# The first expert's w1 split moved into the last router unit, the second w2 load queued behind the first gather, and the first rows split bank by bank

## What is computed

```python
x = attention(q, k, v, cap)              # 4 batches, 12 heads, 448 rows, 64 columns, tanh-capped scores
x = square(relu(x @ w_in)) @ w_out       # 1792 x 768, inner width 2048
# a mixture of 8 experts, each of capacity 224 tokens
logits = x @ w_gate                      # 1792 x 8
order = argsort(-logits.flatten())       # greedy: the best (token, expert) pairs first
for idx in order:                        # a pair is taken if the token is free and the expert not full
    tok, e = idx // 8, idx % 8
    ...
for e in range(8):
    h = maximum(x[assigned == e] @ w1[e], 0)      # w1[e]: 768 x 1024
    out[assigned == e] = h @ w2[e]                # w2[e]: 1024 x 768
```

## Time and profile before

| what | value |
|---|---|
| median of 3 runs | 1215.44 us (1215.41 to 1217.42) |
| the profiled execution | 1214.78 us, its span 1213.0 us |
| PE busy | 1110.7 us, 92% of the span |
| DVE busy | 832.2 us, 69% |
| ACT busy | 623.8 us, 51% |
| POOL busy | 212.3 us, 17% |
| PE's mean granted clock | 0.944 of full speed |

### The profile page before, as it was taken

One profiled execution on the slowest core, in us unless ns is written; L12 is line 12 of the kernel. 1 busy time (PEld: TensorE's weight loads), 2 busy tenths in 40 slices (PEclk: granted clock), 3 DMA queues, 4 the chain that ended last, 5 costly groups with the idle time before them and its releaser, 6 DMA issues.

```text
span 1213.0 us, 25561 instructions
## 1 busy us (share of the span) xinstructions
PE 1110.7 (92%) x9795; PEld 905.9 (75%) x9795; DVE 832.2 (69%) x1741; ACT 623.8 (51%) x977; POOL 212.3 (17%) x345
## 2 busy tenths in 40 slices
PE   6999988999998999999967999999994599999997
PEld 6974434444443999999966999999994588888885
DVE  3159998999999366666574455555556589898972
ACT  1268876999996233333343111111135387878872
POOL 0025444454453000000000000000000022222201
PEclk7569998999999999999987999999996799999999
DMA  7017311111110000000150000000336456666501
GB/s 262 16 50 186 104 45 46 45 54 59 53 31 16 1 2 1 2 2 1 41 170 2 24 25 25 24 2 24 128 128 224 157 213 249 234 247 240 209 24 46
DMA packets 54644, 103.46 MB, mean 85 GB/s; under 512 B 3872, under 2 KB 32288, under 8 KB 54560
## 3 DMA queue, kind: packets, MB, share of 16 engines
q1 hardware_dynamic: 52000, 91.26, 22.2%
q0 software_dynamic: 2560, 11.01, 2.9%
HBM read 91.25 MB, written 11.01 MB: 84 GB/s over the span
## 4 chain that ended last, share of the span: by engine, by line
PE 68%; DVE 15%; ACT 7%; issue 6%; POOL 1%; DMA 1%; DVEq 0%; ACTq 0%; SPq 0%; POOLq 0%
PE psum L1278 17%; PE psum L1319 15%; PE psum L1438 6%; PE psum L1424 6%; PE psum L1204 5%; PE psum L1218 4%; PE psum L1229 4%; PE psum L1188 3%; DVE arena L1116 2%; ACT arena L694 2%; DVE arena L840 2%; PE psum L1362 2%; PE psum L1181 2%; DVE arena L1110 2%; ACT arena L599 2%
## 5 line engine op out<-in xcount | busy, mean ns | idle before, releaser
L1319 PE MATMUL psum<-arena 128*128 128x224 f16 x2304 | 243.2, 261 | 18.1 <-DVE arena L804 18.1
L1319 PEld LDWEIGHTS psum<-arena 128*128 128x128 f16 x2304 | 215.5, 99 | 22.2 <-DVE arena L804 19.0
L1278 PE MATMUL psum<-arena 128*128 128x224 f16 x2304 | 223.3, 259 | 0.0
L1278 PEld LDWEIGHTS psum<-arena 128*128 128x128 f16 x2304 | 220.2, 98 | 2.0 <-ACT arena L616 1.1
L476 POOL TENSOR_SCALAR arena<-arena 112x448 f32<-112x448 f32 x192 | 121.8, 647 | 191.6 <-DVE arena L830 191.6
L599 ACT ACTIVATE arena<-arena 112x448 f32<-112x448 f32 x192 | 143.6, 751 | 4.3 <-DVE arena L842 4.1
L1229 PEld LDWEIGHTS psum<-arena 112*112 112x112 f32 x768 | 74.3, 135 | 87.0 <-POOL arena L476 56.0
L1424 PE MATMUL psum<-arena 128*128 128x224 f16 x1152 | 116.5, 266 | 16.0 <-DVE arena L1124 16.0
L1424 PEld LDWEIGHTS psum<-arena 128*128 128x128 f16 x1152 | 112.9, 100 | 19.8 <-issue 14.1
L1438 PE MATMUL psum<-arena 128*112 128x384 f16 x768 | 127.1, 326 | 0.4 <-issue 0.4
L590 ACT ACTIVATE arena<-psum,arena 112x896 f32<-112x896 f32 x96 | 96.5, 1005 | 51.5 <-PE psum L1204 50.6
(11 more groups left out here) (207 smaller groups left out, 1273.0 us busy)
## 6 DMA issues: line engine op xcount, KB each, us to landing
arena<-moe_w SPq DMA_DIRECT2D x16, 3072.0 KB, 13.4
arena<-moe_w_out SPq DMA_DIRECT2D x32, 384.0 KB, 4.1
arena<-moe_w_in SPq DMA_DIRECT2D x16, 384.0 KB, 5.2
arena<-q SPq DMA_DIRECT2D x24, 224.0 KB, 2.9
arena<-k SPq DMA_DIRECT2D x24, 224.0 KB, 3.1
arena<-v SPq DMA_DIRECT2D x24, 224.0 KB, 2.7
y_rows<-arena SPq DMA_DIRECT2D x16, 336.0 KB, 3.2
arena<-y_rows,arena POOLq DMA_INDIRECT x16, 4.6
```

The lines of the kernel that those rows point to most:

```text
L1278: last = pe.matmul(out, w_split[:, f, z, k * 128:(k + 1) * 128], x[u % 2][:, k, :], start=(k == 0 and m == 0), stop=(k == KD - 1 and m == 2))
L1319: last = pe.matmul(out, w_split[:, k, z, m * 128:(m + 1) * 128], g[u][:, k, :], start=(k == 0 and j == 0), stop=(k == KF - 1 and j == 2))
```

## The change

Five things are done; the first three are one piece.

1. The sums of absolute values of w1 of expert 0 (ACT, four instructions) stand in unit 6, between `y_evict(6, 0)` and `yT_evict(6, 1)`, instead of at the start of unit 7. The scale is made by DVE in the first round of the last router phase.
2. At the start of unit 7 ACT makes the four quarters of the high half.
3. POOL makes the low half: for each quarter a multiplication of the staged float32 words by the scale, in place, and a subtraction of the float16 high half, written as float16.
4. SP waits for the first gather to land before it issues the load of w2 of expert 1.
5. In the tail between unit 7 and the experts, PE ranks before it transposes the last block; DVE makes the small tables before the large one, and the large one in two halves, with PE's product following half by half; `turn_rows` signals each bank; and for expert 0 ACT and DVE split the rows bank by bank. ACT's sums of w2 of expert 0 come ahead of that, right behind the last unit. `gather_rows(e)` and the later experts' wait count three signals for each expert where they counted one.

```diff
             load_w(1, 0, s_w1l, s_w1L, w1p, KD)
+            sp.wait_ge(s_ygl, 32)
+            sp.sem_inc(s_sp, 1)
             load_w(1, 1, s_w2l, s_w2L, w2p, KE)
...
             pool.partition_all_reduce(w1_tops, w1_sums, 128, RMAX).then_inc(s_wt, 1)
+            for j in range(4):
+                quarter = slice(j * EW // 4, (j + 1) * EW // 4)
+                hold(s_w1H, j + 1)
+                stage = stage_part(0, j * EW // 4, EW // 4)
+                pool.tensor_scalar(stage, stage, w1_scl, 1.0, ALU.mult, ALU.mult).then_inc(s_w1s, 1)
+                hold(s_w1s, j + 1)
+                pool.tensor_tensor(w1L[:, quarter], stage, w1H[:, quarter], ALU.subtract).then_inc(s_w1L, 1)
             hold(s_ym, NU)
...
             for u in range(NU):
                 if u == NU - 1:
-                    act.wait_ge(s_w1l, 16)
-                    act.wait_ge(s_ym, NU - 1)
+                    act.wait_ge(s_we1, 3)
                     for j in range(4):
-                        wait(act, s_ws, j)
-                        act.activation(abs_out, stage_part(0, j * EW // 4, EW // 4), ACT.Abs, accum_out=w1_sums[:, j:j + 1]).then_inc(s_ws, 1)
+                        quarter = slice(j * EW // 4, (j + 1) * EW // 4)
+                        act.activation(w1H[:, quarter], stage_part(0, j * EW // 4, EW // 4), ACT.Copy, scale=w1_scl).then_inc(s_w1H, 1)
                 yT_evict(u, 0)
...
                 y_evict(u, 0)
+                if u == NU - 2:
+                    act.wait_ge(s_w1l, 16)
+                    act.wait_ge(s_ym, NU - 2)
+                    for j in range(4):
+                        wait(act, s_ws, j)
+                        act.activation(abs_out, stage_part(0, j * EW // 4, EW // 4), ACT.Abs, accum_out=w1_sums[:, j:j + 1]).then_inc(s_ws, 1)
                 yT_evict(u, 1)
...
-                w1_hi(0)
-                w1_hi(1)
+                if not first(e + 2):
+                    w1_hi(0)
+                    w1_hi(1)
                 rows_out(1)
...
-                w1_hi(2)
                 if first(e + 2):
-                    w1_hi(3)
+                    act.wait_ge(s_ym, NU)
                     for j in range(4):
                         w2_abs(e + 2, j)
-                if expert_live(e + 2):
-                    wait(act, s_tT, e + 3)
+                    ygH_banks = ygH.rearrange("p (b n) -> p b n", b=3)
+                    act.wait_ge(s_we1, 4)
+                    for b in range(2):
+                        act.wait_ge(s_tT, b + 1)
+                        act.activation(ygH_banks[:, b], psum[:, BANK_ET + b, 0:2 * CAP], ACT.Copy, scale=y2_scl).then_inc(s_ygB, 1)
+                    act.wait_ge(s_tT, 3)
+                    act.activation(ygH_banks[:, 2], psum[:, BANK_ET + 2, 0:2 * CAP], ACT.Copy, scale=y2_scl).then_inc(s_ygH, 1)
+                else:
+                    w1_hi(2)
+                if expert_live(e + 2) and not first(e + 2):
+                    wait(act, s_tT, 3 * (e + 3))
...
                     if r > 0:
                         read_count()
+                    elif phase == E - 2:
+                        dve.wait_ge(s_wt, 1)
+                        dve.tensor_reduce(w1_amax, w1_tops, AX.X, ALU.max).then_inc(s_wa1, 1)
+                        dve.wait_ge(s_wa1, 1)
+                        pow2_scale(dve, w1_amax, w1_inv, w1_scl, s_we1, 0)
...
-            dve.tensor_tensor(low_hot[0:TP], low_of[0:TP].unsqueeze(2).broadcast_to([TP, CH, TP]),
-                              lows[0:TP].unsqueeze(1).broadcast_to([TP, CH, TP]), ALU.is_equal).then_inc(s_hot, 1)
...
             dve.tensor_tensor(group_tok[0:TP], group_hot[0:TP], tok[0:TP].unsqueeze(2).broadcast_to([TP, CH, CH]), ALU.mult).then_inc(s_hot, 1)
+            for h in range(2):
+                half = slice(h * CH // 2, (h + 1) * CH // 2)
+                dve.tensor_tensor(low_hot[0:TP, half], low_of[0:TP, half].unsqueeze(2).broadcast_to([TP, CH // 2, TP]),
+                                  lows[0:TP].unsqueeze(1).broadcast_to([TP, CH // 2, TP]), ALU.is_equal).then_inc(s_hot, 1)
...
+                    if first(e):
+                        ygL_banks, ygH_banks = (y.rearrange("p (b n) -> p b n", b=3) for y in (ygL, ygH))
+                        for b in range(3):
...
+                            last = dve.scalar_tensor_tensor(ygL_banks[:, b], psum[:, BANK_ET + b, 0:2 * CAP], y2_scl, ygH_banks[:, b],
+                                                            ALU.mult, ALU.subtract)
+                        last.then_inc(s_ygL, 1)
+                        return
                     w_lo(e, 0, w1H, w1L, w1_scl, s_w1H, s_w1L)
...
-            turn(NU - 1, 2)
             pe.wait_ge(s_pb, 1)
             ranks(psum[0:TP, BANK_POS, 0:CH * E], live_bf[0:TP], E).then_inc(s_pp, 1)
-            pe.wait_ge(s_hot, 2)
+            turn(NU - 1, 2)
             for c in range(CH):
+                if c % (CH // 2) == 0:
+                    pe.wait_ge(s_hot, 2 + c // (CH // 2))
...
                     for c in range(2):
                         last = pe.transpose(psum[:, BANK_ET + k // 2, (k % 2) * CAP + c * TP:(k % 2) * CAP + (c + 1) * TP],
                                             yg[0:TP, c, k * 128:(k + 1) * 128], ident[0:TP, 0:TP])
-                last.then_inc(s_tT, 1)
+                    if k % 2 == 1:
+                        last.then_inc(s_tT, 1)
```

More of the change, by code:

```diff
@@ L236, in build @@
         s_wm2, s_wa2, s_we2, s_w2H, s_w2L = sem("w2_max"), sem("w2_amax"), sem("w2_scale"), sem("w2_hi"), sem("w2_lo")
-        s_tT, s_ygH, s_ygL = sem("rows_transposed"), sem("rows_hi"), sem("rows_lo")
+        s_tT, s_ygH, s_ygL, s_ygB, s_w1s = sem("rows_transposed"), sem("rows_hi"), sem("rows_lo"), sem("first_rows_hi_by_bank"), sem("first_w1_scaled")
         s_E1, s_ER, s_em, s_ea, s_ee, s_eH, s_eL = sem("expert_up"), sem("expert_relu"), sem("eh_max"), sem("eh_amax"), sem("eh_scale"), sem("eh_hi"), sem("eh_lo")
@@ L527, in gather_rows @@
             def gather_rows(e):
-                hold(s_tT, e)
+                hold(s_tT, 3 * e)
                 pool.tensor_copy(row_idx[0:TP], ids[0:TP, bass.ds(2 * e, 2)]).then_inc(s_gidx, 1)
@@ L663, in y_bound @@
                 act.wait_ge(s_yT, 3 * (u + 1))
-                if u == NU - 1:
+                if u == NU - 2:
                     act.wait_ge(s_ws, 4)
@@ L1120, in up_lo @@
                 def up_lo(e):
+                    if first(e):
+                        ygL_banks, ygH_banks = (y.rearrange("p (b n) -> p b n", b=3) for y in (ygL, ygH))
+                        for b in range(3):
+                            if b < 2:
+                                dve.wait_ge(s_ygB, b + 1)
+                            else:
+                                dve.wait_ge(s_ygH, 1)
+                            last = dve.scalar_tensor_tensor(ygL_banks[:, b], psum[:, BANK_ET + b, 0:2 * CAP], y2_scl, ygH_banks[:, b],
+                                                            ALU.mult, ALU.subtract)
+                        last.then_inc(s_ygL, 1)
+                        return
                     w_lo(e, 0, w1H, w1L, w1_scl, s_w1H, s_w1L)
@@ L1140, in step @@
                 if expert_live(e + 2):
[L1141 to L1144, removed]
+                    if not first(e + 2):
                         w_absmax(e + 2, 0, s_w1l, w1_max, s_wm1)
-                    wait(dve, s_wa1, e + 3)
-                    pow2_scale(dve, w1_amax, w1_inv, w1_scl, s_we1, 4 * (e + 2))
+                        wait(dve, s_wa1, e + 3)
+                        pow2_scale(dve, w1_amax, w1_inv, w1_scl, s_we1, 4 * (e + 2))
                 if first(e + 1):
```

## The result

The change makes the kernel slower: 1222.72 us (median of 4 runs, 1221.07 to 1224.88) against 1216.38 us (median of 4, 1215.41 to 1217.42), ratio 1.0053 with a 95% interval of 1.0034 to 1.0072. The forecast was 1219.5 us in a range of 1209 to 1225, with slower as the likeliest way. The kernel before, timed again beside the experiments, lay between 1208.0 and 1218.0 us over 32 runs, with medians of 1213.53 and 1214.84, so a difference of 6.3 us between totals is smaller than what one kernel shows from run to run; what the change does is read from stretches of the trace.

The account below looks back on a forecast made before the run. PE was taken as the bound to 920 us, then a chain of hand-overs: 9.3 us lost in the unit less 5.2 gained in the tail (1.8 + 1.3 + 2.1) is +4.1, giving 1219.5 us, range 1209 to 1225.

Parts of the forecast that it names:

- The obstruction of POOL and DVE: Last router unit: five DVE instructions a search round and POOL's eight wait for each other's whole length, losing 9.3 us.
- The 9.3: Net loss forecast for the last router unit, in us; 3.7 with a short subtraction, 14.9 with a long one.
- my own sum: Last router unit's loss: 21.0 us of alternating work, less PE's work 6.9, DVE's slack 3.4 and first-instruction slack 1.4.
- the alternation: Last router unit: one POOL instruction for each of five DVE instructions a round, POOL's eight lasting 1.6 rounds, 21.0 us.
- the slack subtracted: Search rounds: DVE's slack of 1.4 and 0.73 us a round takes 3.4 us off; the first POOL instruction's slack, 1.4.
- POOL's copy moves from 926.33 to about 924.5: a gain of 1.8: Tail: reordered ranks and tables bring the row numbers' copy forward, capped by the last row stores landing at 924.2.
- The gather: Tail, POOL's copy to PE's transposes: holding w2 of expert 1 makes the first gather land 1.3 us sooner.
- the half that runs first: Gather estimate: half of the competing weight bytes go, said to be the half running first, so 1.3 us was taken.
- the lower bound: Smallest gain considered for the gather in the tail: 0, against an upper bound of 3.4 us.
- Bank by bank: Tail, first transpose to `expert_up(0)`: splitting rows by bank cuts 5.85 us to 3.75, a gain of 2.1.
- the rival with half clock: Router unit: stalls halve PE's clock for 5 to 10 us, 2 to 4 us more, 1222 to 1226; chance 0.13.
- What cost nothing did: ACT's sums and high halves in the router units, and loads held behind the gather, were forecast to cost nothing.

Follow-up runs that it names:

- the first experiment: Changed kernel without POOL's eight instructions, DVE making the low half of w1 behind the token numbers: 1212.85 us, ratio 0.9977 to the kernel before.
- tail alone: Changed kernel with w1's high half (ACT) and low half (DVE) both moved to the tail, sums left in unit 6: 1208.79 us in one run.
- fifth experiment: Kernel with the low half on DVE, plus one one-word elementwise POOL instruction in the last router unit: tail 24.6 us.
- scalings alone: Changed kernel with only the four scalings on POOL and the subtractions on DVE in the tail: unit 35.3 us, tail 23.3 us, one run.

## Why the prediction came out as it did

**The obstruction of POOL and DVE: right, and for the reason given.** Its mark in the trace was as described for DVE, whose instructions took 1 to 3 us; PE waited for the comparisons in two rounds only, and longest at the end of the phase. Each of POOL's eight instructions held up one of DVE's, as the sum had it: 19.8 us from the first start to the last end (forecast 21.0). Cutting POOL's instructions in eighths all but removed the loss. The assumption that a two-input DVE instruction waits for POOL, which the trace of before could not show, held.

**Its size: 9.3 us forecast, 12.4 measured.** The term that was missing is the half clock behind the stalls, which I had kept out of the sum as a rival of 2 to 4 us. The 9.3 stood for waits alone, and PE's waits came to 7.95. With the measured 19.8 us in place of 21.0 my own sum gives 19.8 − 6.9 − 3.4 − 1.4 = 8.1, so the alternation and the slack subtracted were about right. The other 4.45 us are slower matmuls. The instructions themselves were near the forecast: the scaling mostly 1.55 us (1.6), the subtraction 3.1 to 3.4 (3.0; the prediction's estimate from the Trainium skill, GPSIMD Engine Reference, "Performance versus the Vector engine", was 3.4), the eight together 19.2 us of work (18.4). What I had wrong besides is where they fall. I had them start at 889, some 6 us into the unit, and end in the search rounds. They started 15 us into it, and the last three met the chain at the end of the phase: L1048, L1049 and L1077 took 2.26, 1.48 and 2.99 us where PE has nothing in hand, one wait of 5.14 us.

**The switch of POOL's code: missed, and it stood in the trace of before.** Behind attention, the first all-reduce came at 398.35 with 8.88 us of idle time put down to "issue", while its data were ready at 391.8, and the query by its line shows MODIFY_POOL_CONFIG at 392.2:

```profile
398.35 0.38 POOL L499 PARTITION_ALL_REDUCE arena<-arena  x1 [8.88 <-issue]
```

```profile
L499 POOLq MODIFY_POOL_CONFIG  x2: 11/11/11, 392.2 to 392.2; - x2
```

I counted POOL as ready as soon as its inputs were. The step that failed is "POOL's copy moves from 926.33 to about 924.5: a gain of 1.8". After the change it came 8.55 us behind the last down piece, against 8.73 before, a gain of 0.2; in the first experiment, where POOL had no elementwise work, 6.86, which is the 1.8 forecast. The switch alone does not explain the tail, though: where POOL's copy did come 1.7 us earlier than after the change, the tail was shorter by 0.1 us (first experiment, 22.4) or 0.6 (tail alone, 21.9), since a gather issued earlier took longer to land.

**The gather: 1.3 forecast, 0.7 measured** (10.02 us from copy to transposes against 10.75). The experiment with both loads held shows that the load to hold was w1, the one in flight. The prediction let it run for 9 us, to about 931, so that it would have ended while the gather was under way. In the first experiment the view of its DMA issues says how long it took from its issue at 921.92:

```profile
arena<-moe_w SPq DMA_DIRECT2D x1, 3072.0 KB, 15.1
```

After the change it took 14.3 us from 931.36 and landed at about 945.7, just before the transposes at 946.34, so it was in flight for nearly the whole of the gather. With that an earlier copy brings little, as measured, and the gains of 1.8 and 1.3 could not be added as they were. The prediction's sentence calls the bytes that go the half that runs first; w1, which stays, runs first, and by that the value should have been nearer to the lower bound.

**Bank by bank: 2.1 forecast, 1.9 measured**: 950.29 − 946.34 = 3.95 us instead of 5.85.

**Sum.** +12.4 − 0.2 − 0.7 − 1.9 = +9.6 us on unit and tail, of which the rest of the kernel gave 1.1 back and the first stretch of the profiled execution 2.3, which makes the 6.3 between the two spans. The medians are 6.3 apart too; how much of the difference between 9.6 and 6.3 they owe to the first stretch, whose length varies by more than that between executions, the profile of one execution can't say. The forecast of the same stretches was +4.1, less than half: 3.1 us too little in the unit and 2.4 too much in the tail. So that the total came within 3.2 us of the forecast is in part luck, 2.3 us of an earlier start and 1.0 of clock in `expert_up(0)`. The median of 1222.72 lies in the stated range, but just above the forecast's own 1217.5 to 1222.5, in the 1222 to 1226 of the rival with half clock, whose chance was given as 0.13 and whose mechanism was there.

**What cost nothing did**: ACT's sums and high halves in the units (first experiment, unit 34.4; unit 6 34.6 us with the sums, as before), the held loads (rest 270.1 with both held, 270.1 before).

## What to carry to other kernels

Idle time on GpSimd is not free time: before elementwise work goes there, look what VectorE does at that time with two SBUF inputs or from SBUF to SBUF, and compare the length of one GpSimd instruction with the slack of the chain, not their sums of busy time. Where GpSimd alternates between kinds of work, look for idle time before an instruction that is put down to "issue" although its data were there, and keep such a change of kind off a chain of hand-overs. A gather on the critical path is best issued with nothing else in flight: of two loads ahead of it, the one that runs at that moment is the one to hold. And a gain of time ahead of such a gather is not a gain behind it while that load is still running.

## What the hardware showed that I had not expected

- POOL's change from all-reduce to elementwise work took 7.1 to 10.4 us from MODIFY_POOL_CONFIG to the first instruction, the change back 5.7 to 6.2; once (fifth experiment) an indirect DMA behind it was 5.89 us late too.
- A POOL memset of 2.66 us held up DVE's one-input SBUF to SBUF instruction of 0.30 us for its whole length, and its two-input ones not at all.
- DVE's two-input instructions went with a longer making of descriptors on POOL for one indirect DMA: 2.32 us (first experiment) and 2.72 (scalings alone) instead of 1.28. With DVE's work beside it all the same, it took 1.38 in the fifth experiment.
- On POOL 192 words took 0.42 us for a scaling and 0.55 for a subtraction, 1536 words 1.55 and 3.2: 0.84 and 2.0 ns a word behind a fixed 0.26 and 0.17 us, and 0.18 us lie between two that depend on each other. Cutting each instruction in eight therefore doubled the time that the work occupied POOL, from 20 to 39 us.
